# Attention's row maxima turned by one product and laid into rows by two small DMAs per head

## The reference

```python
scores = scale * np.matmul(q, k.transpose(0, 1, 3, 2))      # 32 heads, 576 x 576, head_dim 64
thresh = np.max(scores, axis=-1, keepdims=True) - tau
scores = np.where(scores >= thresh, scores, -1000000000.0)
scores = scores - np.max(scores, axis=-1, keepdims=True)
attn = np.exp(scores)
attn = attn / (np.sum(attn, axis=-1, keepdims=True) + 1e-09)
x = np.matmul(attn, v)                                       # then the experts, then the dense layer
```

## Time and profile before

| | us |
|---|---|
| median of 3 runs | 1330.28 (1329.15 to 1330.89) |
| time of the profiled execution | 1329.52 |
| its span in the profile | 1327.8 |
| TensorE busy in the span | 1261.7 (95%) |
| VectorE busy | 625.0 (47%) |
| ScalarE busy | 535.8 (40%) |
| GpSimd busy | 521.9 (39%) |

### The profile page before, as it was taken

The page is one execution under the profiler, slowest core; times in us unless marked ns, Lnnn a source line. Parts: engine busy times, 40 slices in busy tenths (PEclk is TensorE's granted clock), DMA queues, the critical chain, the costliest instruction groups (busy, mean ns, idle before and its releaser), DMA issues.

```text
span 1327.8 us, 22028 instructions
## 1 busy us (share of the span) xinstructions
PE 1261.7 (95%) x7777; PEld 1148.3 (86%) x7777; DVE 625.0 (47%) x1226; ACT 535.8 (40%) x955; POOL 521.9 (39%) x373
## 2 busy tenths in 40 slices
PE   4999999999984799999999999998999999999998
PEld 3999999999842689989998999997998999899997
DVE  5799888988715211112111111215545535445433
ACT  2688787878742232333333233332222112111211
POOL 0677888778721252543435254355411101000000
PEclk9999999999987799999999999999999999999999
DMA  5555555555320332423333242344311102000000
GB/s 132 121 141 134 131 135 131 136 126 136 121 69 0 103 127 96 158 83 126 126 109 127 95 158 81 126 150 141 98 56 49 48 0 72 16 0 24 16 1 24
DMA packets 112491, 123.63 MB, mean 93 GB/s; under 512 B 56752, under 2 KB 75440, under 8 KB 112432
## 3 DMA queue, kind: packets, MB, share of 16 engines
q1 hardware_dynamic: 98560, 87.70, 24.0%
q0 software_dynamic: 6080, 19.93, 4.7%
q10 hardware_dynamic: 7792, 15.21, 3.2%
HBM read 81.90 MB, written 19.92 MB: 77 GB/s over the span
## 4 chain that ended last, share of the span: by engine, by line
PE 83%; POOL 5%; issue 4%; DVE 3%; ACT 3%; DMA 2%; POOLq 0%; ACTq 0%; SPq 0%; DVEq 0%
PE h_ps L659 32%; PE y_ps L676 10%; PE y_ps L677 10%; PE y_ps L678 10%; PE o_acc L542 6%; POOL probs_lo L1155 3%; PE ring L503 2%; PE ring L504 2%; PE ring L516 2%; PE ring L517 2%; PE t_ps L637 2%; PE logits_t_ps L584 1%; ACT probs_hi L752 1%; PE turned_r L575 1%; PE ring L526 1%
## 5 line engine op out<-in xcount | busy, mean ns | idle before, releaser
L659 PE MATMUL h_ps<-x_hi,region_a 128*128 128x384 f32 (+1 forms) x1408 | 340.2, 314 | 2.9 <-DVE x_lo L1059 2.9
L1155 POOL TENSOR_TENSOR probs_lo<-probs,probs_hi 128x576 fp32r<-128x576 f32 x160 | 226.2, 1427 | 76.8 <-ACT probs_hi L752 76.8
L659 PEld LDWEIGHTS h_ps<-x_hi,region_a 128*128 128x128 f32 x1408 | 244.9, 189 | 8.9 <-DVE x_lo L1059 3.5
L659 PE MATMUL h_ps<-x_lo,region_a 128*128 128x384 f32 (+1 forms) x704 | 219.7, 312 | 0.0
L1069 DVE SCALAR_TENSOR_TENSOR h_lo<-h_ps,h_hi 128x256 fp32r<-128x256 f32 (+1 forms) x128 | 62.8, 491 | 317.5 <-ACT h_hi L837 294.4
L840 ACT ACTIVATE h_hi<-act_out 128x384 fp32r<-128x384 f32 (+1 forms) x112 | 53.7, 479 | 309.6 <-DVE act_out L1078 306.9
L676 PE MATMUL y_ps<-region_b,h_hi 128*128 128x512 f32 x448 | 176.0, 393 | 1.5 <-DVE h_lo L1084 1.5
L677 PE MATMUL y_ps<-region_b,h_hi 128*128 128x512 f32 x448 | 176.3, 393 | 0.0
L678 PE MATMUL y_ps<-region_b,h_lo 128*128 128x512 f32 x448 | 176.0, 393 | 0.0
L1141 POOL TENSOR_TENSOR region_b<-stage,region_b 128x1024 fp32r<-128x1024 f32 x40 | 95.8, 2396 | 167.5 <-ACT region_b L733 167.4
L837 ACT ACTIVATE h_hi<-h_ps 128x256 fp32r<-128x256 f32 (+1 forms) x128 | 56.0, 437 | 242.1 <-PE h_ps L659 235.6
(11 more groups left out here) (166 smaller groups left out, 2396.6 us busy)
## 6 DMA issues: line engine op xcount, KB each, us to landing
stage<-in_moe_w SPq DMA_DIRECT2D x56, 512.0 KB, 3.5
expert_rows<-rows_out ACTq DMA_DIRECT2D x8, 768.0 KB, 3.9
k_ones<-q_hi SPq DMA_DIRECT2D x32, 160.0 KB, 2.7
q_lo<-k_parts SPq DMA_DIRECT2D x32, 160.0 KB, 2.6
q_hi<-q_hi SPq DMA_DIRECT2D x32, 160.0 KB, 2.4
k_parts<-k_ones SPq DMA_DIRECT2D x32, 160.0 KB, 2.7
qk_nat<-in_q SPq DMA_DIRECT2D x32, 128.0 KB, 2.7
qk_nat<-in_k SPq DMA_DIRECT2D x32, 128.0 KB, 2.8
```

What stands on the lines that cost most here:

```text
L659: mm = pe.matmul(h_ps[:, c % 2, 0:width], wt, x[kind][:, cc, :], start=(n == 0), stop=(n == 3 * C - 1))
L1155: pool.tensor_tensor(probs_lo[:, m % 4, :], probs[:, m % 4, :], probs_hi[:, m % 4, :].bitcast(F32), ALU.subtract).then_inc(lo_done, 1)
```

## The change

The ten columns of maxima (five tiles, high and low) stand side by side in one 68-column tile, `max_cols`, and one product turns them into ten rows of 128. VectorE copies the ten rows to SBUF (`max_rows`), and the SP queue lays them end to end into rows 66 and 67 of `q_lo` with two DMAs of 5 x 128 elements. ScalarE's copy is gone. The turning stands in slot 2 instead of 3 (and 7, 12, 17), ahead of PV instead of behind it; the outputs of a head are turned three heads behind instead of two, still behind PV. The output DMAs stand in slots 8 and 18 instead of 4 and 14, and a load of finished outputs near the end of the attention stands two slots later.

```diff
-        max_cols = sb("max_cols", [P, NT, D + 4], F32R)
+        max_cols = sb("max_cols", [P, D + 4], F32R)
+        max_rows = sb("max_rows", [2 * NT, 2, P], F32R)
...
-            return c // NT + 1 if c % NT == 3 else None
+            return c // NT + 1 if c % NT == 2 else None
...
+                g = max_rows_in(i, c)
+                if g is not None and has(i, g, NH, U):
+                    wait(sp, max_moved, head(i, g) + 1)
+                    for n in range(2):
+                        row = D + 2 + n
+                        sp.dma_start(q_lo[row:row + 1, g % U, :].bitcast(F32).rearrange("p (t n) -> p t n", t=NT),
+                                     max_rows[n * NT:n * NT + NT, g % 2, :].bitcast(F32)).then_inc(max_in[g % 2], 16)
...
-                if c in (NT - 1, 3 * NT - 1) and has(i, c // NT - 1, NH, U):
-                    h = c // NT - 1
-                    wait(sp, freed, past("om", i, h + 2))
+                if c in (NT + 3, 3 * NT + 3) and has(i, c // NT - 2, NH, U):
+                    h = c // NT - 2
+                    wait(sp, freed, past("om", i, h + 3))
...
                     if j == 0:
-                        wait(pe, max_in, head(i, c // NT) + 1)
-                        wait(pe, max_tail_in, head(i, c // NT) + 1)
+                        g = c // NT
+                        wait(pe, max_in[g % 2], (head(i, g - g % 2) // 2 + 1) * 32)
...
+                f = max_rows_in(i, c)
+                if f is not None and has(i, f, NH + 3, U):
+                    place_free(pe, "om", i, f)
+                if f is not None and has(i, f, NH, U):
+                    wait(pe, max_split, head(i, f) + 1)
+                    pe.matmul(ring[0:D + 4, place("om", i, f), 1, 0:P], max_cols[:, :], ident_r[:, :], start=True, stop=True).then_inc(max_turned, 1)
...
-                    for t in range(FULL):
-                        mm = pe.matmul(at[0:D + 4, 1, t * P:t * P + P], max_cols[:, t, :], ident_r[:, :], start=True, stop=True)
-                    mm = pe.matmul(at[0:D + 4, 0, MAX_TAIL:MAX_TAIL + TAIL], max_cols[:, FULL, :], ident_r[:, 0:TAIL], start=True, stop=True)
-                    mm.then_inc(max_turned, 1)
-                if f is not None and has(i, f - 2, NH, U):
-                    h = f - 2
+                if f is not None and has(i, f - 3, NH, U):
+                    h = f - 3
...
-                if f is not None and has(i, f, NH, U):
-                    wait(act, max_turned, head(i, f) + 1)
-                    act.activation(q_lo[D:D + 4, f % U, 0:FULL * P], ring[D:D + 4, place("om", i, f), 1, :], ACT.Copy).then_inc(max_in, 1)
...
-                    dve.tensor_copy(q_lo[D:D + 4, f % U, FULL * P:S],
-                                    ring[D:D + 4, place("om", i, f), 0, MAX_TAIL:MAX_TAIL + TAIL]).then_inc(max_tail_in, 1)
-                    wait(dve, max_in, head(i, f) + 1)
+                    wait(dve, max_in[f % 2], head(i, f - f % 2) // 2 * 32)
+                    dve.tensor_copy(max_rows[:, f % 2, :], ring[0:2 * NT, place("om", i, f), 1, 0:P]).then_inc(max_moved, 1)
```

More of the change, by code:

```diff
@@ L108, in build @@
         s_ready = sem("s_ready"); freed = sem("freed"); max_split = sem("max_split"); max_hi = sem("max_hi")
-        max_turned = sem("max_turned"); max_in = sem("max_in"); max_tail_in = sem("max_tail_in")
+        max_turned = sem("max_turned"); max_in = [sem(f"max_in{i}") for i in range(2)]; max_moved = sem("max_moved")
         st_ready = sem("st_ready"); exp_done = sem("exp_done")
@@ L274, in build @@
         FIRST = -14
-        LAST = TILES + NT
+        LAST = TILES + NT + 4
         WHOLE = (B - 1) * S // P
-        MAX_TAIL = 384
         SPLIT_AT = (5, 10)
@@ L320, in build @@
             for kind, m, total in (("s", n + AHEAD, TILES), ("st", n, TILES), ("qk", -1 if g is None else n // SL * U + g, NH),
-                                   ("om", -1 if f is None else n // SL * U + f, NH + 2)):
+                                   ("om", -1 if f is None else n // SL * U + f, NH + 3)):
                 if 0 <= m < total:
@@ L437, in slot_and_rows @@
                 slot(i, c)
-                for k, (n, heads) in enumerate(((TILES - 8, NH - H), (TILES - 3, NH - 2))):
+                for k, (n, heads) in enumerate(((TILES - 8, NH - H), (TILES - 1, NH - 2))):
                     if isinstance(i, int) and tile(i, c) == n:
@@ L446, in _ @@
             slots(sp, slot_and_rows)
-            sp.wait_ge(freed, past("om", 0, NH + 1))
+            sp.wait_ge(freed, past("om", 0, NH + 2))
             for s in x_out:
@@ L544, in slot @@
                     mm.then_inc(pv_done, 1)
-                f = max_rows_in(i, c)
-                if f is not None and has(i, f, NH + 2, U):
-                    place_free(pe, "om", i, f)
-                if f is not None and has(i, f, NH, U):
-                    at = ring[:, place("om", i, f)]
-                    wait(pe, max_split, head(i, f) + 1)
-                    for t in range(FULL):
-                        mm = pe.matmul(at[0:D + 4, 1, t * P:t * P + P], max_cols[:, t, :], ident_r[:, :], start=True, stop=True)
-                    mm = pe.matmul(at[0:D + 4, 0, MAX_TAIL:MAX_TAIL + TAIL], max_cols[:, FULL, :], ident_r[:, 0:TAIL], start=True, stop=True)
-                    mm.then_inc(max_turned, 1)
-                if f is not None and has(i, f - 2, NH, U):
-                    h = f - 2
+                if f is not None and has(i, f - 3, NH, U):
+                    h = f - 3
                     wait(pe, ot_out, head(i, h) + 1)
@@ L565, in _ @@
             x_early = early[:, :].rearrange("p (t d) -> p t d", d=DM)
-            pe.wait_ge(freed, past("om", 0, NH + 1))
+            pe.wait_ge(freed, past("om", 0, NH + 2))
             pe.wait_ge(route_in, 48)
@@ L791, in _ @@
             slots(act, slot)
-            act.wait_ge(freed, past("om", 0, NH + 1))
+            act.wait_ge(freed, past("om", 0, NH + 2))
             def copy_logits(g):
@@ L894, in _ @@
             dve.memset(q_lo[D:D + 4, :, :].bitcast(F32), 0.0)
-            dve.memset(max_cols[:, :, 0:D + 2].bitcast(F32), 0.0)
+            dve.memset(max_cols[:, :].bitcast(F32), 0.0)
             dve.memset(o_t[:, :, :], 0.0)
@@ L921, in slot @@
                     whole = neg_max[:, g % 2, :, 0:1].bitcast(F32)
-                    dve.tensor_reduce(max_cols[:, :, D + 2:D + 3], whole, AX.X, ALU.max)
+                    dve.tensor_reduce(max_cols[:, 0:NT].rearrange("p (t o) -> p t o", o=1), whole, AX.X, ALU.max)
                     dve.tensor_reduce(neg_max[:, g % 2, :, 1:2], whole, AX.X, ALU.max, negate=True).then_inc(max_hi, 1)
@@ L934, in slot @@
                     wait(dve, max_hi, head(i, g) * 2 + 2)
-                    dve.tensor_reduce(max_cols[:, :, D + 3:D + 4], max_rest[:, :].rearrange("p (t o) -> p t o", o=1),
+                    dve.tensor_reduce(max_cols[:, NT:2 * NT].rearrange("p (t o) -> p t o", o=1), max_rest[:, :].rearrange("p (t o) -> p t o", o=1),
                                       AX.X, ALU.max).then_inc(max_split, 1)
@@ L945, in slot @@
                     wait(dve, max_turned, head(i, f) + 1)
-                    if has(i, f - 2, NH, U):
-                        wait(dve, o_turned, head(i, f - 2) + 1)
-                    dve.tensor_copy(q_lo[D:D + 4, f % U, FULL * P:S],
-                                    ring[D:D + 4, place("om", i, f), 0, MAX_TAIL:MAX_TAIL + TAIL]).then_inc(max_tail_in, 1)
-                    wait(dve, max_in, head(i, f) + 1)
-                    if not has(i, f - 2, NH, U):
+                    wait(dve, max_in[f % 2], head(i, f - f % 2) // 2 * 32)
+                    dve.tensor_copy(max_rows[:, f % 2, :], ring[0:2 * NT, place("om", i, f), 1, 0:P]).then_inc(max_moved, 1)
+                    if not has(i, f - 3, NH, U):
+                        dve.wait_ge(max_moved, head(i, f) + 1)
                         dve.memset(den[:, :], 0.0).then_inc(freed, 1)
-                if f is not None and has(i, f - 2, NH, U):
-                    h = f - 2
+                if f is not None and has(i, f - 3, NH, U):
+                    h = f - 3
+                    if has(i, f, NH, U):
+                        dve.wait_ge(max_moved, head(i, f) + 1)
                     wait(dve, o_turned, head(i, h) + 1)
@@ L1163, in _ @@
             slots(pool, slot)
-            pool.wait_ge(freed, past("om", 0, NH + 1))
+            pool.wait_ge(freed, past("om", 0, NH + 2))
             float_iota = lambda out, pattern, **k: pool.iota(out, pattern, allow_small_or_imprecise_dtypes=True, **k).then_inc(route_pool, 1)
```

## The result

The changed kernel takes 1339.01 us (median of 4 runs, 1337.38 to 1341.33), the kernel before 1329.88 (4 runs on the same chip). The ratio is 1.0069, with a 95% interval of 1.005 to 1.0088: 9.1 us slower. One run of all that follow, 1367.39 us in experiment 7 at a lower granted clock, is left out of its ratio. The profiled execution took 1337.81 us, its span is 1336.1, which is 8.3 more than before.

What follows compares the result with a forecast made beforehand. TensorE (PE), busy for 95% of the span, was taken as the bound. 12.0 - 2.9 + 3.4 = +12.5 us on 1329.52 made 1342.0; with the runs' median 0.8 above, 1342.5 was given, range 1327 to 1351.

Steps and rivals of the forecast that it cites:

- the chain: From q/k turning in slot 16 through SP's queue to ST of slot 5: 2.0 us later in six rounds, 12.0 us.
- the other heads: Two heads in each of seven rounds keep the saved products' 0.21 us: 2.9 us less, bounds 0 and 4.2.
- the clock: PE's granted clock falls after the new wait in two of six rounds, 1.7 us each: 3.4 us more.
- the end of the attention: Last heads, where PE already waits for GpSimd: the saving there was counted at nothing.
- The last addition of the prediction: From 1342.0 for the profiled execution, with the median of runs 0.8 above it, to the 1342.5 given.
- The shift on SP: Output DMAs ahead of the loads of q and k delay SP's queue by 1.8 us, bounds 1.6 and 2.0.
- The small DMAs: Two DMAs of maxima behind L408 in slot 1: 0.6 us of SP each, landing 2.1 us after issue.
- the doubt about the ring: Waits around the new product in slot 2 and ST of slot 3: 0.3 to 0.4 us could eat the 0.21.
- the maxima are in time: Rival, chance 0.17: no wait at ST of slot 5, saved products make it faster, 1326 us.
- Late in all heads: Rival, chance 0.13: slow landing of 3.7 us, ST of slot 5 3.6 late, slot 15 0.7; 1353 and more.

Runs made afterwards that it cites:

- experiment 7: Kernel before, with one product of the maxima written beside ST of slot 2, two small DMAs, outputs in old slots: 1327.86 us, ratio 0.9992.
- experiment 1: Changed kernel with its output DMAs behind the seven loads again, in slots 4 and 14, one pair later than before: 1328.3 us, ratio 0.9997.
- experiment 6: Changed kernel with a third DMA of 5 x 128 elements, to an unread spare tile, ahead of the two: 1348.21 us, ratio 1.014.
- experiment 4: Changed kernel with the two DMAs of maxima issued from ScalarE's queue in slot 3 instead of SP: 1340.4 us, ratio 1.0086.
- experiment 2: Kernel before, with only its output DMAs moved from slots 4 and 14 to 8 and 18: 1333.71 us, ratio 1.0035.
- experiment 3: Changed kernel without the two DMAs of maxima and the waits for them, row maximum left out of ST: 1331.49 us, ratio 1.0014.
- experiment 5: Changed kernel with one DMA of 10 x 128 elements for both rows of maxima instead of two: 1335.0 us, ratio 1.0044.

## Why the prediction was right, and where its numbers were off

It was right in sign, place and mechanism: 1342.5 forecast, 1339.0 measured, inside the range of 1327 to 1351 and the forecast's own of 1337 to 1349. Experiment 1 shows the cause by undoing it alone. The profiled execution has 8.3 us more where the sum had 12.5. The difference is made of the chain (+1.2), the other heads (+0.5), the clock (-3.4), the end of the attention (-2.75) and the rest (+0.3). The last addition of the prediction is off by 0.3 besides: 1342.0 and 0.8 make 1342.8. By its steps:

- **The shift on SP** was 1.8, and L408 of slot 1 came 1.80 us later. The first load came 3.1 behind the last DMA of slot 18 (2.8 to 3.2 was given).
- **The small DMAs** take the queue for 1.5 us together, which is 0.15 a piece more than the 0.6 assumed, and ST starts about 1.9 behind the second one (issued 0.8 behind the first, as in experiment 6, where the rows stand apart: 216.94 + 0.8 to 219.61). The issues were 0.2 dearer in all and the landing 0.2 shorter than the 2.1 assumed, so the two errors cancel. The second DMA was issued 7.8 behind the turning of slot 1, with 7.9 forecast. The Trainium skill, "DMA: Bandwidth & Descriptors", section "Anatomy of one DMA", has a fixed part of about 2.0 us for a DMA, whatever its size. It gives this for DMAs that GpSimd issues; these come from SP, and with 2.5 KB each the 1.9 us are near it. The 5.6 us at the end of experiment 4 are far above it.
- **The chain** grew by 2.2 in six rounds, not by 2.0: 13.2 against 12.0.
- **The heads outside the chain** gave back 2.4 in the rounds, and 2.9 was forecast with those of a seventh round. Two heads in six rounds at 0.21 are 2.5. That this fits is luck: the doubt about the ring was justified in every head, with 0.2 to 0.3 us lost around the product. Outside the chain it went unseen, because waits of PV for GpSimd of 0.27 and 0.41 went at the same time, which the prediction did not have. Inside the chain no such wait was there and it costs 0.5 a round (experiment 1), which does not show as long as SP holds ST.
- **The clock** was the mis-sized term: 3.4 forecast, 0 in the profiled execution. It was 1.00 in all six rounds, through idle stretches of 1.15 to 1.61 us. That execution is one of the two faster of four (1337.38 and 1337.81, mean granted clock 0.983). The slower two (1340.21 and 1341.33) have 0.980, and 0.003 x 1336 = 4.0 us, an estimate, is about all that divides them from the others. Where the clock fell in them no profile shows, and runs of the kernel before spread as well, from 0.978 to 0.984. The ground for it was weak, too: the idle of 1.34 near 356 us, which I took as what lowered the clock, is there again in experiment 2, and there the clock stays at 1.00.
- **The end of the attention** was counted at nothing and gave 2.75. Before, the granted clock over this stretch was 0.95, after it is 1.00: 0.05 x 55.65 = 2.8 us by itself. But experiment 2 has 1.00 as well and still needs 54.8, 0.5 of it one more wait for a DMA, while the kernels with the product as a use of its own in slot 2 and outputs three heads behind (the changed one, experiments 1, 3, 5 and 6) need 52.7 to 53.0. Experiment 4 is built so too, but has the late landing shown there. In the changed kernel PE waits for GpSimd 1.4 us in this stretch instead of 4.8. By that, 1.3 (55.65 to 54.3) would be the clock's and 1.4 that wait's, but the two were not separated by a run of their own.

The stretch before the change with all engines in windows, and PE's wait for GpSimd in it; the changed kernel and then experiment 2 with PE in windows, the latter with the same wait:

```profile
320.84:376.49 55.65, 48.70 (x364) 46.02 (x363) 38.67 (x80) 39.66 (x72) 42.28 (x33) 0.95 0.43 129
```

```profile
PE o_acc L542 <- POOL probs_lo L1155: 4.8, 7, 1.3
```

```profile
331.58:384.48 52.90, 47.85 (x353) 1.00 0.43 126
```

```profile
325.98:380.80 54.82, 47.14 (x364) 1.00 0.46 137
```

```profile
PE o_acc L542 <- POOL probs_lo L1155: 5.0, 7, 1.3
```

- **Not seen at all** was the second reader of the late queue, S of slot 7. It costs nothing in the changed kernel as timed, but it would take 3.2 us of what one hopes to regain by speeding up the maxima alone. It is the larger part of why experiment 3 did not come below the kernel before.

Of the rivals, "the maxima are in time" is what experiment 1 brings about. Its 1326 was too low, since the rounds gain only outside the chain. "Late in all heads" came about with one more small DMA (experiment 6), though by the queue and not by a slow landing. A landing behind a large load that was slower than the rival's 3.7 shows once only, at the end of experiment 4.

## What to carry to other kernels

A queue that issues back to back is a serial engine. Before something is put ahead of something else on it, list every reader behind that place with the slack of each, and not only the one for which the change is made: here there were three (ST of slot 5 with none, S of slot 7 with 1.2 us, ST of slot 15). Small DMAs count by their number, at 0.7 to 0.8 us of queue each, and moving them to a compute engine's queue moves the price to whatever waits on that engine. Two queues also have no order between them: from the second queue the small DMAs came behind a large load that they had stood ahead of. When several small uses of a shared ring are merged, look at what waits around the merged one in every head: here 0.2 to 0.3 us around a product of 0.06 ate its saving, and in half of the heads it only took the place of another wait. Letting it ride beside ST took those waits away, but the time fell below that of the kernel before only with one small DMA less.

## What the runs showed of the hardware that was not expected

- Issuing a DMA of 2.5 KB takes 0.7 to 0.8 us of SP and 0.72 of ScalarE, no less than one of 160 KB (L421, 0.60).
- A pair of 2.5 KB DMAs issued about 1 us behind a load of 3328 KB on another queue was waited for until 5.6 us after the second issue, with the DMA engines busy throughout (experiment 4, share 1.00 and 363 GB/s from 364 to 370 us). In the loops it was 1.9.
- TensorE's granted clock stayed at 1.00 (2.4 GHz) through six idle stretches of 1.15 to 1.61 us in otherwise dense work, and fell in three rounds of experiment 6, where they were 1.56 to 2.10. In that kernel's other three rounds those ahead of slot 5 were 0.78 to 1.34. The ranges of the two kernels overlap. An idle of 1.34 us stood beside a lower clock in one kernel and beside 1.00 in another. The length of one idle stretch alone does not tell whether the clock falls.
